# First MLP: two groups of 768 tokens with seven block products each, in place of the last four groups of 384

## What is computed

```python
scores = np.matmul(q_c, k_c.transpose(0, 1, 2, 4, 3)) / np.sqrt(64)
attn = softmax(scores)                     # over the 64 keys of the chunk
x = np.matmul(attn, v_c)                   # -> (2304, 512)
h = x @ w1;  g = h - np.tanh(h);  x = g @ w1_out          # first MLP
h = x @ w2;  sp = np.log1p(np.exp(h));  g = h * np.tanh(sp)
out = g @ w2_out                                          # second MLP
```

## Time and profile before

| | |
|---|---|
| median of 3 runs | 824.29 us (824.09 to 824.30) |
| the profiled execution: own time, span | 823.91 us, 822.1 us |
| TensorE busy | 812.8 us (99%) |
| VectorE busy | 543.9 us (66%) |
| ScalarE busy | 361.9 us (44%) |
| GpSimd busy | 150.5 us (18%) |
| DRAM traffic | 91.49 MB read, 35.91 MB written |

### The profile page before, as it was taken

The page is one execution under the profiler, slowest core; times in us unless marked ns, Lnnn a source line. Parts: engine busy times, 40 slices in busy tenths (PEclk is TensorE's granted clock), DMA queues, the critical chain, the costliest instruction groups (busy, mean ns, idle before and its releaser), DMA issues.

```text
span 822.1 us, 13517 instructions
## 1 busy us (share of the span) xinstructions
PE 812.8 (99%) x5394; PEld 765.6 (93%) x5394; DVE 543.9 (66%) x819; ACT 361.9 (44%) x567; POOL 150.5 (18%) x213
## 2 busy tenths in 40 slices
PE   7999999999999999999999999999999999999998
PEld 6999999999999999999999889888988988888896
DVE  6766555655555655534447788888877777877775
ACT  4544433343344344333335455546445435445434
POOL 4322244334415413410110111110000000000000
PEclk9999999999999999999999999999999999999999
DMA  7653355444425434422654265397424276523302
GB/s 242 210 177 99 101 186 193 133 159 180 168 74 198 157 115 157 179 65 90 231 194 164 90 231 192 129 354 311 153 92 177 90 272 236 195 90 127 143 0 77
DMA packets 41597, 132.21 MB, mean 161 GB/s; under 512 B 7104, under 2 KB 10944, under 8 KB 41536
## 3 DMA queue, kind: packets, MB, share of 16 engines
q1 hardware_dynamic: 29088, 83.38, 28.2%
q0 software_dynamic: 12448, 47.98, 16.6%
HBM read 91.49 MB, written 35.91 MB: 155 GB/s over the span
## 4 chain that ended last, share of the span: by engine, by line
PE 91%; DVE 5%; ACT 2%; issue 1%; DMA 0%; SPq 0%
PE psum L945 8%; PE psum L946 8%; PE psum L944 8%; PE psum L931 8%; PE psum L932 7%; PE psum L933 7%; PE psum L1080 7%; PE psum L1081 7%; PE psum L1079 7%; PE psum L1058 6%; PE psum L1059 6%; PE psum L1057 6%; PE psum L892 1%; PE psum L858 1%; PE psum L978 1%
## 5 line engine op out<-in xcount | busy, mean ns | idle before, releaser
L673 DVE TENSOR_TENSOR pool_words<-psum,pool_words 128x384 f32<-128x384 f32 x96 | 53.4, 557 | 120.3 <-ACT pool_words L466 120.3
L946 PE MATMUL psum<-g_hi,w_lo 128*128 128x384 f32 x384 | 128.4, 334 | 0.0
L945 PE MATMUL psum<-g_lo,w_hi 128*128 128x384 f32 x384 | 128.3, 334 | 0.0
L944 PE MATMUL psum<-g_hi,w_hi 128*128 128x384 f32 x384 | 128.3, 334 | 0.0
L931 PE MATMUL psum<-x_hi,w_hi 128*128 128x384 f32 x360 | 122.2, 340 | 0.7 <-DVE w_lo L606 0.7
L932 PE MATMUL psum<-x_lo,w_hi 128*128 128x384 f32 x360 | 120.4, 334 | 0.0
L933 PE MATMUL psum<-x_hi,w_lo 128*128 128x384 f32 x360 | 120.3, 334 | 0.0
L466 ACT ACTIVATE pool_words<-psum 128x384 f32<-128x384 f32 x96 | 46.9, 489 | 146.3 <-PE psum L933 144.3
L1058 PE MATMUL psum<-w_lo,w_hi 128*128 128x384 f32 x288 | 97.5, 339 | 0.0
L1059 PE MATMUL psum<-w_hi,w_lo 128*128 128x384 f32 x288 | 97.0, 337 | 0.0
L1057 PE MATMUL psum<-w_hi 128*128 128x384 f32 x288 | 96.3, 334 | 0.0
(11 more groups left out here) (110 smaller groups left out, 1532.1 us busy)
## 6 DMA issues: line engine op xcount, KB each, us to landing
w_hi<-s_hi SPq DMA_DIRECT2D x24, 896.0 KB, 4.6
w_lo<-s_lo SPq DMA_DIRECT2D x24, 896.0 KB, 6.8
pool_words<-w_out POOLq DMA_DIRECT2D x32, 256.0 KB, 3.8
w_hi<-t_hi SPq DMA_DIRECT2D x18, 384.0 KB, 4.9
w_lo<-t_lo SPq DMA_DIRECT2D x18, 384.0 KB, 5.6
pool_words<-w POOLq DMA_DIRECT2D x24, 256.0 KB, 3.7
pool_words<-qT SPq DMA_DIRECT2D x18, 256.0 KB, 3.8
pool_words<-kT SPq DMA_DIRECT2D x18, 256.0 KB, 5.1
```

Of the source, the lines that this page charges most:

```text
L944: pe.matmul(ps, w_hi[:, 1, cols], g_hi[:, s, :], start=f == 0, stop=False)
L945: pe.matmul(ps, w_hi[:, 1, cols], g_lo[:, s, :], start=False, stop=False)
L946: mm = pe.matmul(ps, w_lo[:, 1, cols], g_hi[:, s, :], start=False, stop=f == FT - 1)
```

## The change

Groups 0 and 1 stay as they are (`PLAIN = 2`). Groups 2 to 5 become two groups of 768 tokens, whose first layer is done with the seven block products (16 pairs q, `mlp1_pair`), and whose second layer (`y1_wide`) has its 768 columns as one matmul of 512 and one of 256, each three times for the halves. The operands for it are made as steps too: eight more weight triples (weight pairs j = 0 to 7 are w1, 8 to 15 w2), stored to `s_hi`/`s_lo` and read back in each pair. The token sums of the first MLP are made straight into SBUF (`add_x`, `x1_hi`, `x1_lo`). Step buffers, source buffers and the places of steps change. The second MLP's pairs stay, save for its first ones, and the splits of w2_out go by two at places in pairs 10 to 15 and in the second MLP's pairs 0 to 2.

The core of the diff (the four sums of `add_weights` each wait for the one before):

```diff
-def block_at(g):
...
-STEPS = (WEIGHT_STEPS[:10] + token_steps(0) + WEIGHT_STEPS[10:23] + token_steps(1) + WEIGHT_STEPS[23:] + token_steps(2))
-SLOTS = (2, 3, 4, 6, 7, 8, 9, 11, 12, 13)
-STEP_AT = {(1 + _k // len(SLOTS), SLOTS[_k % len(SLOTS)]): _k for _k in range(EARLY_STEPS)}
+PLAIN = 2
+PAIRS1 = (SUPERS - 1) * PAIRS
+ORDER1 = (M1, M2, M6, M7, M4, M5, M3)
+BLOCK_BEHIND = {0: 12, 2: 13, 3: 14, 4: 15, 5: 16, 6: 17}
+STEPS_AFTER = {1: (0, 0, 0, 0, 1, 1, 2), PAIRS + 1: (2, 2, 0, 0, 1, 1, 2)}
+STEPS_BESIDE_PAIR = (1, 1, 1, 1, 1, 1, 2)
+STEPS_BESIDE_BLOCK = (1, 1, 0, 0, 1, 1, 1)
+place_steps([("group", 0, f) for f in (12, 13, 14)], weight_steps(0))
+place_steps([("group", 1, f) for f in range(1, 13)], [step for j in range(1, 5) for step in weight_steps(j)])
+place_steps([(1, 1), (1, 2), (1, 3)], _T0[0:3])
+place_steps([(2, 1), (2, 2), (2, 3)], [_T0[3], weight_steps(5)[0], _T0[4]])
+place_steps([(3, 1), (3, 2), (3, 3)], [weight_steps(5)[1], _T0[5], weight_steps(5)[2]])
+place_steps([(4, 0), (4, 1), (4, 2), (4, 3)], [_T0[6]] + weight_steps(6))
+place_steps([(5, 1), (5, 2), (5, 3)], weight_steps(7))
+place_steps([(6, 1), (6, 2), (6, 3)], weight_steps(8))
+place_steps([(PAIRS, 3), (PAIRS + 1, 1), (PAIRS + 1, 2), (PAIRS + 1, 3)], weight_steps(9)[0:2] + [_T1[0], weight_steps(9)[2]])
+for _i in range(1, 7):
+    place_steps([(PAIRS + 1 + _i, r) for r in range(4)], [_T1[_i]] + weight_steps(9 + _i))
+STEP_BUFFER = [1 if what == "weights" and i == 1 and n > 0 else 0 for what, n, i in STEPS]
+RAW_BUFFER = [1, 0, 1, 0, 1] + [0] * 11
+X_SPLIT_AT = {(PAIRS - 1, 1): 0, (PAIRS - 1, 2): 1, (PAIRS - 1, 3): 2, (PAIRS, 0): 3, (PAIRS, "w0"): 4, (PAIRS, 1): 5, (PAIRS, 2): 6}
...
+            def add_weights(j):
+                a22, a11, a12, a21 = (raw[RAW_BUFFER[j]][:, i * BLOCK:(i + 1) * BLOCK] for i in range(4))
+                pool.tensor_tensor(a22, a21, a22, ALU.add).then_inc(weight_sums, 1)
...
             def store_step(k):
                 what, n, i = STEPS[k]
+                pool.wait_ge(step_lo_done, k + 1)
                 if what == "tokens":
+                    if i + 1 < len(TOKEN_STEPS):
+                        add_tokens(n, i + 1)
                 else:
+                    if i == 0:
+                        add_weights(n)
+                pool.dma_start(to_hi, from_hi.bitcast(f32)).then_inc(step_stored[STEP_BUFFER[k]], 16)
+                pool.dma_start(to_lo, from_lo.bitcast(f32)).then_inc(step_stored[STEP_BUFFER[k]], 16)
...
             def step_hi(k):
+                stored = earlier(STEP_BUFFER, k)[0]
+                if stored > 0:
+                    act.wait_ge(step_stored[STEP_BUFFER[k]], 32 * stored)
+                act.activation(step_halves(k)[0], step_source(k), ACT.Copy).then_inc(step_hi_done, 1)
...
 @block.scalar
...
+            def mlp1_pair(q):
+                if q - 1 in BLOCK_BEHIND and BLOCK_BEHIND[q - 1] + 1 < TILES:
+                    exps(BLOCK_BEHIND[q - 1] + 1)
+                beside_pair_hi(q, 0)
+                keep_m1_1(q)
...
+                if q > 0:
+                    hi1(2 * q - 1)
+                beside_pair_hi(q, "w0")
+                if q == PAIRS + 1:
+                    keep_wide_y(0)
+                for r in range(1, 4):
+                    beside_pair_hi(q, r)
+                beside_pair_hi(q, "w1")
+                tanh1(2 * q)
+                hi1(2 * q)
+                tanh1(2 * q + 1)
+                if q in BLOCK_BEHIND:
+                    keep_x(BLOCK_BEHIND[q])
...
 @block.vector
...
+            def mlp1_pair(q):
+                if scored < TILES:
+                    shift(scored)
+                if q > 0:
+                    minus1(2 * q - 1)
+                beside_pair_lo(q, 0)
+                if q > 0:
+                    lo1(2 * q - 1)
+                take1_c11(q)
+                beside_pair_lo(q, "w0")
+                take1_u2(q)
+                if scored < TILES:
+                    normalise(scored)
+                beside_pair_lo(q, 1)
+                take1_u3(q)
+                if scored < TILES:
+                    turn_blocks(scored)
+                if q == PAIRS + 1:
+                    keep_wide_y(0)
+                beside_pair_lo(q, 2)
+                take1_c21(q)
+                beside_pair_lo(q, 3)
+                take1_c22(q)
+                beside_pair_lo(q, "w1")
+                minus1(2 * q)
+                take1_c12(q)
+                lo1(2 * q)
...
 @block.tensor
...
+            def product1(q, place):
+                if q > 0 and place in (4, 5):
+                    pe.wait_ge(sums1_taken, 6 * q + place - 2)
+                if place == 6:
+                    pe.wait_ge(sums1_taken, 6 * q + 5)
...
+                for k in range(HALF_K):
+                    pe.matmul(ps, a_hi, t_hi_words[:, k, :], start=first, stop=False, skip_group_check=i in (M5, M3))
+                    pe.matmul(ps, a_hi, t_lo_words[:, k, :], start=False, stop=False, skip_group_check=i in (M5, M3))
+                    mm = pe.matmul(ps, a_lo, t_hi_words[:, k, :], start=False, stop=end, skip_group_check=i in (M5, M3))
+            def y1_wide(u, j):
+                pe.matmul(bank[j], w_hi[:, 1, at], u_hi[:, 0:512], start=start, stop=False)
+                pe.matmul(bank[j], w_hi[:, 1, at], u_lo[:, 0:512], start=False, stop=False)
+                pe.matmul(bank[j], w_lo[:, 1, at], u_hi[:, 0:512], start=False, stop=end)
+                pe.matmul(half_bank, w_hi[:, 1, at], u_hi[:, 512:WIDE], start=start and j % 2 == 0, stop=False, skip_group_check=True)
+                pe.matmul(half_bank, w_hi[:, 1, at], u_lo[:, 512:WIDE], start=False, stop=False, skip_group_check=True)
+                pe.matmul(half_bank, w_lo[:, 1, at], u_hi[:, 512:WIDE], start=False, stop=end, skip_group_check=True).then_inc(y1_step, 1)
...
+            def mlp1_pair(q):
+                for place in range(7):
+                    product1(q, place)
+                    for _ in range(after[place]):
+                        if q > 0:
+                            y1_wide(*steps.pop(0))
+                if t is not None:
+                    wait_for_values(t)
+                    pe.wait_ge(sums1_taken, 6 * (q + 1))
+                    values(t)
+                for u, j in steps:
+                    y1_wide(u, j)
```

More of the change, by code:

```diff
@@ new lines, with unit_tile, earlier @@
+RAW_BUFFER = [1, 0, 1, 0, 1] + [0] * 11
+X_SPLIT_AT = {(PAIRS - 1, 1): 0, (PAIRS - 1, 2): 1, (PAIRS - 1, 3): 2, (PAIRS, 0): 3, (PAIRS, "w0"): 4, (PAIRS, 1): 5, (PAIRS, 2): 6}
+W2_OUT_AT = {(PAIRS + 2, "w0"): 0}
+for _i in range(5):
+    W2_OUT_AT[PAIRS + 3 + _i, "w0"], W2_OUT_AT[PAIRS + 3 + _i, "w1"] = 2 * _i + 1, 2 * _i + 2
+LATE_SPLIT_AT = {0: (11, 12), 1: (13, 14), 2: (15,)}
+def unit_tile(u):
+    return (u // 2) % PAIRS + (0 if u % 2 else PAIRS)
+def earlier(buffers, n):
+    same = [i for i in range(n) if buffers[i] == buffers[n]]
+    return len(same), same[-1] if same else None
@@ L78, in build, with stores_through @@
+def stores_through(n, buffer):
+    return sum(1 for b in STEP_BUFFER[:n + 1] if b == buffer)
 def build(nc, qT, kT, v, w1, w1_out, w2, w2_out, out):
@@ L387, in _ @@
             load_v(2, v_loaded_2)
-            for t in range(GROUP_TILES, TILES):
+            for t in range(GROUP_TILES, 13):
                 sp.wait_ge(scores_ready, t)
@@ L515, in mlp1_group @@
                         split_chunk_hi(f + 2)
-                    if (g, f) in STEP_AT:
-                        step_hi(STEP_AT[g, f])
-                    if last and f > LAST_LAG:
-                        split_w2_out_hi(f - LAST_LAG - 1)
-                split_g_hi(FT * g + FT - 1)
-                if not last:
-                    tanh(FT * (g + 1))
+                    if ("group", g, f) in STEP_AT:
+                        step_hi(STEP_AT["group", g, f])
+                    if g == 1 and f >= FT - 3:
+                        for place in ((0, 1), (2, 3), (4,))[f - FT + 3]:
+                            x1_hi(0, place)
@@ L536, in _ @@
             tanh(0)
-            for g in range(GROUPS):
+            for g in range(PLAIN):
                 mlp1_group(g)
+            x1_hi(0, 5)
+            for q in range(PAIRS1):
+                mlp1_pair(q)
             def u_exp(u):
@@ new lines, in mlp1_pair @@
+            def mlp1_pair(q):
+                t = BLOCK_BEHIND.get(q)
+                steps = [(u, j) for u in (2 * q - 3, 2 * q - 2) if u >= 0 for j in range(KT)]
+                after = STEPS_AFTER.get(q, STEPS_BESIDE_BLOCK if t is not None else STEPS_BESIDE_PAIR)
+                for place in range(7):
+                    product1(q, place)
+                    if q == 0 and place == 5:
+                        y1(PLAIN - 1, FT - 4)
+                    for _ in range(after[place]):
+                        if q > 0:
+                            y1_wide(*steps.pop(0))
+                if q == 0:
+                    y1(PLAIN - 1, FT - 3)
+                if t is not None:
```

(12 more changed lines are left out.)

709 lines of the change are left out of this document (450 added, 259 removed).

## The result

| | before | after |
|---|---|---|
| median of 6 runs each | 824.28 us (823.94 to 824.46) | 1031.46 us (1025.97 to 1033.90) |
| TensorE busy | 812.8 us (99%) | 860.1 us (83%) |
| DRAM traffic | 91.49 MB read, 35.91 written | 125.04 MB read, 50.59 written |

The ratio is 1.2508 (95% interval 1.2478 to 1.2537): 207 us slower, where I had 125, and past the top of my range (1000). The runs of the changed kernel lie up to 8 us apart, so two single runs of this family are told apart only beyond that.

The account below looks back on a forecast made before the run. TensorE's instruction stream was taken as the bound; after the change, 808.1 + 118.5 staging + 4 group 1 + 2 seams + 14 clock = 947 us of span, 949 us as run. Range 922 to 1000, or 875 to 1000 down to the third rival.

Parts of the forecast that it names:

- +4: Group 1: step stores for weight parts 0 and 2 run late against the hidden tiles, costing 4 us.
- Staging chain, +118.5: Sixteen pairs: operand steps wait for stores in one shared buffer, holding the takes and then TensorE; +118.5 us.
- the seams: Two places where the output layer's banks are copied with only 3.15 us of products between: +2 us.
- TensorE's stalls thin out the other transfers: Reason for taking store landings near the quiet end, 3.6 us for 384 KB and 2.8 for 256 KB.
- The clock, +14: Pairs: work right behind TensorE's idle gaps starts at the low clock level; +14 us, bounds 0 and 25.
- TensorE's own gain, -14.0: Block products in the hidden layer save 15.2 us, 512- and 256-column output matmuls add 1.2; net -14.0 us.
- TensorE stays the bound: Rival for the whole kernel: staging fits the slack, 812 us, faster by 1.5%; chance 0.03.
- Staging is hidden, but the ordering DMAs are not: Rival: ordering DMAs cost 18 us, giving 830, or 256-column loads give 833; chance 0.05.
- Only the leg inside a pair costs: Rival: nine pairs x 4.2 us and about 35 in pairs 1, 2, 3, 9 give 885; chance 0.20.
- The low clock holds throughout: Rival: C to U doubles, pairs 2 to 6 +50 and 10 to 15 +34, giving 1019; chance 0.10.
- the signs promised: High halves waiting over 100 us for s, t stores; M5's take awaited; pairs 10 to 15 every 22 to 25 us.

Follow-up runs that it names:

- e2: Changed kernel without the eight ordering DMAs of each attention tile from the fourth on; values wait only for VectorE's block transposition: 988.0 us.
- e5: Changed kernel with both no ordering DMAs and no wait of early steps' high halves for stores, save those of the first weight triple: 912.8 us.
- e7: e5 with only two of the w2_out pieces loaded and the first two slot loads one block later: 891.8 us.
- e8: e7 with the four weight sums, and the waits for them, also left out: 862.5 us.
- e4: Changed kernel with step buffers as if always free: early high halves wait for no store, save those of the first weight triple: 966.7 us.
- e9: Changed kernel with 28 unread matmuls of 128 columns ahead of the seventh product in twelve pairs, to keep TensorE at work: 1030.6 us.

## Why the prediction was wrong

**The step that failed is the term for groups 0 and 1: "+4", a stall of step stores in group 1.** Measured it is +70.8 (208.9 less the 138.1 of TensorE's own work there), 40.8 of them the ordering DMAs by e2, then, in this order of taking away, 1.8 with the buffers (e5), 7.0 with the loads that e7 changes, 4.5 with the sums (e8). Of the 16.7 that e8 still has, 6.0 and 4.9 are the two gaps read there; about 6 are open. The stall that I had named, of step stores in group 1, is worth those 1.8 at most: with the stores out of the way and the ordering in place (e4) the groups took 209.1. I costed the ordering DMAs (5.57 us and 1.9) for pairs 3 to 6 alone and never followed them in the plain groups, because the text of the change says that those groups stay as they are. They do, but for `BLOCK_AT`: since the pairs offer six places behind them for blocks, nine blocks must stand in groups 0 and 1, at two or three tiles' distance. The ring's length could have been read from the trace of before: from a block's scores over its division, turn, ordering and landing to its values, 17.7 us with `y1`, against the blocks' new distance of 13.7 or less. That comparison was missing. (The 1.9 us of the earlier trace rows are also the median of single DMAs from their own issue; the last of a tile landed 1.2 to 3.4 us after the queue was done issuing.)

**Staging chain, +118.5:** right in mechanism, near in size for the pairs as a whole: with the clock and the seams the forecast loses 134.5 us there, and measured are 406.7 - 255.6 = 151.1. The experiments give the store waits 67.4 of these (e4) and the sums 28.9 (e7 to e8). Another 11.4 are the ordering (e4 to e5) and 13.2 the loads (e5 to e7), which I had put at nothing; 30 are open, with the clock in them. Pair by pair, forecast against the distance of starts: pairs 1 to 3 28.0, 29.1 and 25.8 against 28.3, 32.8 and 27.4 (28.0 is pair 1's own 11.6, with one output unit, and 16.4); pairs 4 to 6 25.6 (the prediction adds 8.75 to 16.8 and writes 26.3) against 30.1, 27.3, 26.9; 7 and 8 15.8 against 16.2 and 15.9; 9 24.0 against 26.8; 10 to 15 together 140.1 against 157.4. The mis-sized term is the landing of a token store in the pairs of four steps: 3.6 us taken, 6.9, 6.2, 4.5, 8.4, 6.6 and 9.9 measured (mean 7.1), so 3.5 x 6 = 21 us against the 17 that these pairs are longer. "TensorE's stalls thin out the other transfers" was the reason for the low value; but each pair still loads a slot of 1.8 MB, and its longer chain only shifts the store into it. The weight stores there landed in 2.6 to 4.7, and in 4.2 to 6.7 in pair 15; 3.6 and 2.8 had been taken.

**The clock, +14:** borne out in size where it can be read, 2.2 and 2.3 us in pairs 2 and 3 by e9 where 2.5 was forecast; the sum over all pairs is not shown, since e9's fillers held up eight of them. In the plain groups, which I had left out, it is a link of the ring: 4.1 us for `y1` instead of 2.1. The Trainium skill's "TensorE: Matmul & The Clock Gate", section "HAM oscillation — how this bites in real kernels", says that in the kernel it describes each wait between bursts returns the clock to half; the granted clock of 0.84 in both stages, and of 0.50 to 0.72 in the stretches behind the seventh product of pairs 2 to 6 and 9 to 15, agrees.

**TensorE's own gain, -14.0:** confirmed in its prices. The wide output step from the timeline of the changed kernel:

```profile
554.30 0.40 PE L1358 MATMUL psum<-x_hi,w_lo 128*128 128x512 f32 x1
554.53 0.27 PE L1360 MATMUL psum<-x_hi,w_hi 128*128 128x256 f32 x1
554.64 0.28 PE L1361 MATMUL psum<-x_lo,w_hi 128*128 128x256 f32 x1
554.76 0.28 PE L1362 MATMUL psum<-x_hi,w_lo 128*128 128x256 f32 x1
554.88 0.34 PE L1337 MATMUL psum<-w_hi 128*128 128x384 f32 x1
```

A 256-column matmul is 0.11 to 0.12 us (0.118 taken), one of 512 columns 0.23. The last stage is 397.1 against 395.0 by my terms. The two seams are in pairs 1 and 9, with a wait of 2.1 us each; I had taken 2 for both.

**The rivals.** "TensorE stays the bound" is refuted by 172 us of idle TensorE. "Staging is hidden, but the ordering DMAs are not" had the second cause and gave it 18 us, in the pairs alone and instead of staging; both came true together, and that combination had no place in my cases. "Only the leg inside a pair costs", 885, is refuted by the pairs' 406.7 us. "The low clock holds throughout", 1019, is near the result for a wrong reason. Of the signs promised, pairs 10 to 15 came later than said (24.2 to 26.4 us and, the last, 30.6, not 22 to 25); the others were there (M5's take, high halves waiting over 100 us for the s and t stores, 145 measured), and none of them could show what was left out.

**Range.** Its ends moved only staging and clock terms. The ordering, at its price of 18 us in the pairs, would have taken the upper end to 1018, still short: what was missing was its price in the groups. Two slips change nothing: by its terms the lower end is 926, not 922, and the first rival's 812 is 1.2% faster, not 1.5%.

## What to carry to other kernels

Where a change crowds work into fewer places, list everything whose distance to the next of its kind shrinks, and compare each such ring's length (from one instance through all engines and queues to the next) with the new distance, in the stages that "stay as they are" first. A chain that never appears among the waits is not free; it has a slack, which has to be measured before it is spent. When two stalls lie in different stages their costs add, whatever hides what within one.

## What the runs showed of the hardware

- Eight DMAs of 32 KB inside SBUF took SyncE's queue 4.95 to 5.4 us to issue in groups 0 and 1 of the changed kernel, and the last landed 1.2 to 4.1 us after that, so a 256 KB rearrangement was 6.2 to 9.5 us of latency.
- A store of 384 KB landed in 3.3 us with no slot load beside it and in 8.4 with one; loads of 256 KB behind a slot load of 1.8 MB took 10.0 and 10.8 us.
- Twelve matmuls of 384 columns behind a gap took 4.1 us instead of 2.1. Behind the seventh product of a pair, the same work took 8.9 us at a granted clock of 0.71 and 6.7 at 1.00. Matmuls put into the gap to hold the clock gained that only where they were shorter than the gap.
